# Retention with stacked output products in two chunks, small zero products first, a tile moved ahead of an output, and fewer loads under way

## The reference, cut to what matters

```python
gamma = 1.0 - 2.0 ** (-5.0 - np.arange(H))
Dmat = np.where(rel >= 0, gamma[:, None, None] ** rel, 0.0)       # rel = pos_i - pos_j
attn = np.matmul(q @ k.T / 8 * Dmat, v)                            # per batch and head
x = attn.transpose(0, 2, 1, 3).reshape(1152, 512)
for e in range(4):                                                 # moe: D 512, F 1024
    out += p[:, e:e+1] * (np.maximum(x @ w1[e], 0) @ w2[e])
h = out @ w_in                                                     # 512 -> 2048
y = (h * np.tanh(softplus(h))) @ w_out                             # 2048 -> 512
```

## Time and profile before

| what | value |
|---|---|
| median of 3 runs | 619.76 us (619.45 to 620.73) |
| profiled execution | 620.43 us, of which the span from the first to the last instruction 618.7 us |
| PE busy | 606.0 us, 98% of the span |
| DVE, ACT, POOL busy | 262.9, 234.8, 278.3 us |
| DMA moved | 50.47 MB, mean 82 GB/s |
| mean granted TensorE clock | 0.994 |
| chain that ended last | PE 97%, issue 1%, DVE 1%, DMA 1% |

### The profile page before, as it was taken

The page is one execution under the profiler, slowest core; times in us unless marked ns, Lnnn a source line. Parts: engine busy times, 40 slices in busy tenths (PEclk is TensorE's granted clock), DMA queues, the critical chain, the costliest instruction groups (busy, mean ns, idle before and its releaser), DMA issues.

```text
span 618.7 us, 9829 instructions
## 1 busy us (share of the span) xinstructions
PE 606.0 (98%) x4016; PEld 546.6 (88%) x4016; DVE 262.9 (42%) x361; ACT 234.8 (38%) x434; POOL 278.3 (45%) x230
## 2 busy tenths in 40 slices
PE   7799999999999999999999999999999999999997
PEld 4688999999899999999999999989989999989996
DVE  2468654424254424154534154535545432324334
ACT  2466333322233322223432223435455454334431
POOL 3558645534435545335553435532446543443300
PEclk9799999999999999999999999999999999999999
DMA  8963312322102332012332102321211232201002
GB/s 339 334 218 103 87 41 65 119 84 68 35 35 68 104 103 68 35 35 68 103 88 66 52 34 69 103 68 46 58 34 58 67 101 83 68 1 52 1 1 102
DMA packets 24923, 50.47 MB, mean 82 GB/s; under 512 B 2864, under 2 KB 2992, under 8 KB 24880
## 3 DMA queue, kind: packets, MB, share of 16 engines
q1 hardware_dynamic: 24736, 49.84, 25.5%
q10 hardware_dynamic: 144, 0.02, 0.0%
HBM read 47.49 MB, written 2.36 MB: 81 GB/s over the span
## 4 chain that ended last, share of the span: by engine, by line
PE 97%; issue 1%; DVE 1%; DMA 1%; ACT 0%
PE bank L494 31%; PE bank L496 31%; PE bank L495 31%; PE bank L442 2%; PE bank L470 1%; DMA loaded<-in_first 1%; PE bank L474 1%; PE bank L612 1%; PE bank L447 0%; PE bank L619 0%; DVE acc_sb L889 0%; DVE acc_sb L893 0%; ACT st L686 0%; DVE h_lo L850 0%; ACT h_hi L717 0%
## 5 line engine op out<-in xcount | busy, mean ns | idle before, releaser
L395 POOL TENSOR_TENSOR w_lo<-w_raw,w_hi 128x512 fp32r<-128x512 f32 x96 | 133.9, 1409 | 148.4 <-ACT w_hi L368 144.9
L494 PE MATMUL bank<-w_hi,h_hi 128*128 128x512 f32 x432 | 168.7, 390 | 0.0
L496 PE MATMUL bank<-w_hi,h_lo 128*128 128x512 f32 x432 | 168.4, 390 | 0.0
L495 PE MATMUL bank<-w_lo,h_hi 128*128 128x512 f32 x432 | 168.3, 390 | 0.0
L876 DVE TENSOR_TENSOR h_act<-part,bank 128x384 f32<-128x384 f32 x96 | 52.9, 551 | 170.4 <-PE bank L496 169.9
L390 POOL TENSOR_TENSOR ws<-ws_f,ws 128x1024 fp32r<-128x1024 f32 x24 | 58.4, 2432 | 144.7 <-ACT ws L364 144.7
L496 PEld LDWEIGHTS bank<-w_hi,h_lo 128*128 128x128 f32 x432 | 81.1, 188 | 16.9
L495 PEld LDWEIGHTS bank<-w_lo,h_hi 128*128 128x128 f32 x432 | 81.1, 188 | 12.3
L494 PEld LDWEIGHTS bank<-w_hi,h_hi 128*128 128x128 f32 x432 | 81.0, 188 | 12.1
L722 ACT ACTIVATE part<-bank 128x384 f32<-128x384 f32 x72 | 35.4, 491 | 138.9 <-PE bank L496 138.9
L843 DVE SCALAR_TENSOR_TENSOR h_lo<-h_act,h_hi 128x384 fp32r<-128x384 f32 x64 | 73.4, 1156 | 20.9 <-ACT h_hi L712 20.3
(11 more groups left out here) (88 smaller groups left out, 863.8 us busy)
## 6 DMA issues: line engine op xcount, KB each, us to landing
w_raw<-in_weights SPq DMA_DIRECT2D x144, 256.0 KB, 2.8
loaded<-in_toks SPq DMA_DIRECT2D x9, 512.0 KB, 6.4
loaded<-in_feats SPq DMA_DIRECT2D x8, 512.0 KB, 5.9
out<-acc_sb SPq DMA_DIRECT2D x6, 256.0 KB, 2.0
out<-acc_sb SPq DMA_DIRECT2D x1, 768.0 KB, 3.5
loaded<-in_first SPq DMA_DIRECT2D x1, 726.0 KB, 4.4
ident<-in_ident SPq DMA_DIRECT2D x1, 64.0 KB, 6.0
p_nat<-in_probs ACTq DMA_DIRECT2D x1, 18.0 KB, 6.4
```

Of the source, the lines that this page charges most:

```text
L395: pool.tensor_tensor(w_lo[layer][:, x], w_raw[:, r % RAW], w_hi[layer][:, x].bitcast(F32), ALU.subtract).then_inc(s_wl, 1)
L494: pe.matmul(out, w[0], x[0], start=first, stop=False, **more)
L495: pe.matmul(out, w[0], x[1], start=False, stop=False, **more)
L496: return pe.matmul(out, w[1], x[0], start=False, stop=last, **more)
```

## The change

**Stacked outputs** in chunks 1 and 2 (`STACKED`): state and v stand above one another in the 128 partitions, and q and masked scores too, so that one product over 128 rows replaces two over 64. An output then has 16 products and not 32. For this the host gives feats of these chunks with the halves arranged otherwise, DVE multiplies v of batch 1 by its decay into a tile of its own (`v_decay_again`, `s_va`), POOL's `v_decay` covers half the partitions, the state copy of ACT writes into the place below or above v, and masking is two instructions of 64 partitions. **Zeros:** 60 products of 128x64 by 64 columns (`small_zeros`) stand in place of 7 of 128x512. **Tile 0** runs between `scores_and_state(3)` and `output(3)`; `TILES_IN` then has one tile each at chunks 3 to 6, and two at 7. **Loads:** up to chunk 4 each load waits for an earlier one to land, so that at most three are under way. On DVE, `first_lo(c - 2)` stands ahead of `decayed(c - 1)` in chunks 2 and 3.

```diff
+STACKED = 1, 2
-TILES_IN = {3: (0,), 4: (1,), 5: (2, 3), 6: (4,), 7: (5, 6), 8: (7,)}
+TILE_AMID = {3: 0}
+TILES_IN = {3: (1,), 4: (2,), 5: (3,), 6: (4,), 7: (5, 6), 8: (7,)}
...
-WARM_START, WARM_NEXT = 7, 5
+SMALL, WARM_NEXT = 60, 5
...
+        v_again = sb("v_again", [P, len(STACKED), HEADS, DH])
...
+        def state_and_v(c, b):
+
+            return v_again[:, c - 1] if b else slots[:, c % SLOTS, 2]
+
+        def q_and_masked(c, b):
+
+            return slots[:, c % SLOTS, 1 - b]
...
+            load_feats(1)
             for c in range(1, SLOTS):
-                load_feats(c)
+                feats_there(c - 1)
                 load_toks(c)
+                if c + 1 < SLOTS:
+                    toks_there(c - 1)
+                    load_feats(c + 1)
...
                 sp.wait_ge(s_o, c - SLOTS + 1)
+                if c == SLOTS:
+                    feats_there(c - 1)
                 load_feats(c)
+                if c == SLOTS:
+                    toks_there(c - 1)
                 load_toks(c)
...
                 pe.wait_ge(s_vd, c + 1)
+                if c in STACKED:
+                    pe.wait_ge(s_va, c)
...
+            def of_both(c, b, h):
+                return pe.matmul(ps_o[HALF[h % 2], b, h // 2], state_and_v(c, b)[:, h], q_and_masked(c, b)[:, h],
+                                 start=True, stop=True)
...
+                if c in STACKED:
+                    pe.wait_ge(s_xt, c)
+                    pe.wait_ge(s_st, 2 * c)
+                    pe.wait_ge(s_sm, c + 1)
+                    for hp in range(PAIRS):
+                        for b in range(BATCH):
+                            of_both(c, b, 2 * hp)
+                            mm = of_both(c, b, 2 * hp + 1)
+                    mm.then_inc(s_o, 1)
+                    return
...
+            def small_zeros(count):
+
+                for _ in range(count):
+                    pe.matmul(banks[7][HALF[0], 0:CH], zeros[:, 0:CH], zeros[:, 0:CH], start=True, stop=True)
+
             pe.wait_ge(s_zt, 1)
-            keep_warm(WARM_START)
+            small_zeros(SMALL)
...
                     scores_and_state(c)
+                if c in TILE_AMID:
+                    early_tile(TILE_AMID[c])
                 output(c)
...
+                if c + 1 in STACKED:
+                    act.wait_ge(s_va, c + 1)
                 for b in range(BATCH):
-                    act.activation(st[HALF[b], c % 2], ps_state[HALF[1 - b]], ACT.Copy).then_inc(s_st, 1)
+                    to = state_and_v(c + 1, b)[HALF[1 - b]] if c + 1 in STACKED else st[HALF[b], c % 2]
+                    act.activation(to, ps_state[HALF[1 - b]], ACT.Copy).then_inc(s_st, 1)
...
+            def v_decay_again(c):
+
+                dve.wait_ge(s_toks[c % SLOTS], landed(c))
+                by = key_decay[HALF[1], c].unsqueeze(2).broadcast_to([CH, HEADS, DH])
+                dve.tensor_tensor(v_toks(c, 1), slots[HALF[1], c % SLOTS, 2], by, ALU.mult).then_inc(s_va, 1)
...
+                if 1 < c <= PER_BLOCK:
+                    first_lo(c - 2)
                 if c > 0:
                     decayed(c - 1)
-                if c > 1 and c != PER_BLOCK + 1:
+                if c == 1:
+                    v_decay_again(2)
+                if c > PER_BLOCK + 1:
                     first_lo(c - 2)
```

More of the change, by code:

```diff
@@ L512, in plain_ready, with early_tile @@
                     pe.wait_ge(s_cc, ITEMS * (sums(s) - 1) + (C21, C12)[i] + 1)
+            def early_tile(t):
+                s, i = divmod(t, ITEMS)
+                plain_ready(s, i)
+                plain_products(s, i, range(KT))
             def plain_products(s, i, tiles):
@@ L812, in masked @@
                 dve.wait_ge(s_sc, c + 1)
-                dve.tensor_tensor(masked_scores(c), ps_s[c % SCORES], mask.unsqueeze(1).broadcast_to([P, HEADS, CH]),
-                                  ALU.mult).then_inc(s_sm, 1)
+                if c in STACKED:
+                    for b in range(BATCH):
+                        op = dve.tensor_tensor(masked_scores(c, b), ps_s[c % SCORES][HALF[b]],
+                                               mask[HALF[b]].unsqueeze(1).broadcast_to([CH, HEADS, CH]), ALU.mult)
+                    op.then_inc(s_sm, 1)
+                    return
+                dve.tensor_tensor(slots[:, c % SLOTS, 0], ps_s[c % SCORES],
+                                  mask.unsqueeze(1).broadcast_to([P, HEADS, CH]), ALU.mult).then_inc(s_sm, 1)
+            def v_decay_again(c):
+                dve.wait_ge(s_toks[c % SLOTS], landed(c))
+                by = key_decay[HALF[1], c].unsqueeze(2).broadcast_to([CH, HEADS, DH])
+                dve.tensor_tensor(v_toks(c, 1), slots[HALF[1], c % SLOTS, 2], by, ALU.mult).then_inc(s_va, 1)
             def rows(i):
@@ L1028, in v_decay @@
                 pool.wait_ge(s_toks[c % SLOTS], landed(c))
[L1029 to L1030 removed]
+                rows = HALF[0] if c in STACKED else slice(0, P)
+                v = slots[rows, c % SLOTS, 2]
+                by = key_decay[rows, c].unsqueeze(2).broadcast_to([rows.stop, HEADS, DH])
+                pool.tensor_tensor(v, v, by, ALU.mult).then_inc(s_vd, 1)
             pool.wait_ge(s_feats[0], landed(0))
@@ L1078 @@
     weights = [halves(moe_w1[e], moe_w2[e]) for e in range(MOE_EXPERTS)] + [halves(moe2_w_in, moe2_w_out)]
-    feats = np.stack([by_features(k), by_features(q)], axis=3).reshape(PLACES, P, 2 * KIND)
+    feats = np.stack([by_features(k), by_features(q)], axis=3)
+    for c in STACKED:
+        feats[c] = np.stack([feats[c, 1, :, ::-1], feats[c, 0]])
+    feats = feats.reshape(PLACES, P, 2 * KIND)
     toks = np.stack([by_tokens(v), by_tokens(k)], axis=3).reshape(PLACES, P, 2 * KIND)
```

44 lines of the change are left out of this document (25 added, 19 removed).

## The result

| | before | with the change |
|---|---|---|
| median (11 runs each) | 620.02 us (619.19 to 620.88) | 624.17 us (621.42 to 625.38) |
| profiled execution, its span | 620.43, 618.7 us | 624.44, 622.3 us |
| mean granted clock | 0.994 | 0.989 |

The ratio is 1.0053 (95% interval 1.0042 to 1.0064); the two medians lie 4.15 us apart, 0.67%. So the change is slower by 0.5 to 0.7%, where 617.5 us had been forecast, and the time lies above the forecast's range (615.8 to 620.2).

A forecast was written before the change was run, and what follows sets the result against it. PE, 98% busy, bounds the kernel; only early idle time and slow clock could go. Block times gave 2.0 to 3.5 us gain, idle time 0.6 to 2.1; taking 2.2, 619.76 - 2.2 = 617.5 us, 80% range 615.8 to 620.2.

The forecast's parts named there:

- The reading of the gaps: PE's early issue gaps (2.63, 1.24, 1.53, 0.41 us): PE runs out of program at every 256th instruction, its packet late.
- that rival: Small zeros at the start end late, 107 ns each, 2.5 us late on everything: 620.5 us; chance 0.13.
- The start of tile 0: Ahead of output 3, tile 0 waits for DVE's low half of chunk 2 and starts at 23.0 us.
- The loads held back cost nothing.: Loads up to chunk 4: waiting is free while the DMA engines always have a load waiting.
- About 1 us if the last part lags: Held-back loads: cost about 1 us if the last of a load's 16 parts lags, as when a program packet shares its engine.
- A product over 128 rows holds two quarters: Outputs of chunks 1 and 2: PE time stays 0.9 us each, while 64 records go in each chunk.
- The next has one tile and not two: 38.4, or 39.9 if it is late again.: Later block, at 41.88 us before: one tile, 4.1 us, PE goes on at 38.4, or 39.9 if the packet is late.
- A block costs 4.25 to 5.2 us: Early chunks: each 256-instruction block costs PE at least this while DMA engines are full, so fetch paces chunks without a tile.
- Stacked outputs: Chunks 1 and 2: 128 records fewer, later block starts; DVE's four extra operations of 0.6 to 0.7 us hide.
- the zeros: Start: 106 more records bring the third block's request forward to about 6.5 us; the 2.63 us gap goes.
- Tile 0 ahead of output 3: PE idles 1.8 us before tile 0, yet reaches output(4) at 29.9 us with two tiles done, against 30.83 with one.
- The rival of the rule: Early gaps are not due to instruction count, so fewer and earlier records buy nothing: 619.9 us; chance 0.05.

The follow-up runs named there:

- before_small: Kernel before with 60 small zero products in place of 7 large ones, nothing else: 628.12 us against 620.18, ratio 1.0112.
- loads_free: Changed kernel with the loads issued without waiting, as before the change: 621.89 us against 620.18 for the kernel before, ratio 1.0027.
- free_late_weights: loads_free with the weights behind ident issued only when output 5 is done: 621.20 us against 619.76 for the kernel before, ratio 1.0012.
- small_split: before_small with the weights of chunks 5 to 8 issued half a chunk later: 626.38 us against 620.37 for the kernel before, ratio 1.0089.
- before_held: Kernel before with the change's waits ahead of the loads, nothing else: 621.06 us against 620.18, ratio 1.0013.

## Why the prediction was wrong

**What held.** The reading of the gaps as a program that comes late in blocks of 256 instructions: they moved where the count had put them, near 14 us there is none, and the gap at the last records of `scores_and_state(2)` ended at 18.27 (17.8 forecast). The small zeros took 57 ns each (3.41 us for 60; 53 in before_small with 3.17) and ended ahead of the first load, so that rival fell. (The 0.43 us of a large one is 0.45, 3.17 by seven, and the gaps of 6.3 us are 6.0 by the earlier trace rows; neither changes the forecast.) The start of tile 0 was right for a kernel with free loads (22.97, 23.0 forecast). That there is no gap near 14 was partly luck: two of the three kernels with the same records and free loads have one.

**The step that failed first: "The loads held back cost nothing."** It had a condition, that the DMA engines always have a load waiting and that a load moves within 1.5 us of its issue. From 10.6 to 20.8 us they moved 231 to 284 GB/s, against 399 to 410 with free loads; toks 3 took 6.89 us, not the 4 that three loads of 1.3 us would. "About 1 us if the last part lags" was right in kind and too small, for what it delays was not followed: two weights on SP, then ACT's queue, where a high half of a weight stands ahead of the state copy and of `xa_hi`, then DVE, tile 0, and the whole of tile 0 and `output(3)` at 1.2 GHz. Measured 2.3 us by the medians (loads_free; 1.6 by the ratios), and 0.9 in the kernel before.

**The second: "A product over 128 rows holds two quarters, so 32 passes of it last as long as 64 passes over four quarters: 0.9 us of PE time stay."** That is about right for the output itself (1.15 us for `output(1)` after; 1.1 for an output of 64 passes before, 42.45 to 43.55). But the sum has `scores_and_state(1)` at 1.0 us and puts nothing for what the turned features do to it and to `scores_and_state(0)`: they take 2.0 and 1.9 us, 2 us of PE time more. It put the costs of stacking on DVE, and took PE as unchanged.

**"The next has one tile and not two: 38.4, or 39.9 if it is late again."** In loads_free, free of the waits, PE goes on at 41.80 where before did at 41.88, and its packet lies at 39.4 us, as before at 39.3. All that had been won by then was lost in a gap of 2.20 us, which the double tile had covered before. The forecast had named the mechanism (a burst of loads ahead of the packet) and given it 1.5 us; PE went on 3.4 us later than 38.4.

**"A block costs 4.25 to 5.2 us"** was taken as a price of the block. It is a price of the place. before_small asks for the same blocks of the same work at other moments and has gaps of 3.23, 2.88, 1.78 and 3.56 us. That the loads issued just ahead of the request set it fits free_late_weights (from 4.2 to 1.1 us between the entry and the packet), the one run that holds back nothing but such a burst. But that is one crossing in one trace of each, packets of the same program start up to 2 us apart, the medians don't tell the two apart, and small_split left 6 us of the 8. So this is likely, and not shown. What is shown is the size, up to 8 us by a shift of 106 records, and that it lies in the time until the packet starts.

**"Stacked outputs" and "the zeros"** were costed as parts that hold on their own, with two sums that agreed on 2.0. Both came from one model of the fetch and so could not support one another. Alone, one costs 2.5 us and the other 8. Together with the old tiles and free loads they end at 620.70, no change from before (0.9992 to 1.0018).

**"Tile 0 ahead of output 3"** was included at its gaps (1.8 us idle, one double tile fewer) and expected to come out ahead at the later block. It is a loss of 1.2 to 1.3 us in both kernels in which it was varied alone.

**Outside the span** nothing had been foreseen. Kernels with stacked chunks have 2.1 us there (624.44 - 622.3; 621.81 - 619.7; 622.48 - 620.4), those without 1.8 (621.07 - 619.3; 619.66 - 617.8). The cause is open; it is 0.3 of the 4 us.

**The rival of the rule** gave 619.9 and did not come about: before_small has 11.5 us of gaps at crossings. The page "Runtime: NRT & Kernel Launch" of the Trainium skill, section "Instruction fetch mechanics", calls the cost of a crossing "mostly hidden"; the 11.5 us speak against that for this stretch. The blocks of 256 instructions that the Trainium skill states there agree with the records counted in all sixteen traces.

In terms of the sum, by the medians: loads +2.3 us where 0 had been put, tile +1.2 where it was thought to pay, stacking, zeros and DVE's order together +0.5 (within the noise of 0) where 2 to 3.5 of gain had been put, with what lies outside the span inside these. They add up to 4.0 by the way they are formed, run by run from the changed kernel to the kernel before, so that this is no check of them; by the ratios they are 0.26, 0.22 and 0.05%.

## What to carry to other kernels

Where a profile shows gaps of "issue" at every 256th instruction while loads run, count where the boundaries fall before and after any edit that changes the number of instructions, and measure several shifts of a few dozen cheap instructions: here a shift moved the time from -0.1% to +1.1%, more than any part of the change was meant to bring. An edit that adds or removes instructions can't be judged alone in such a stretch, only beside a run that keeps the count. When data is laid out anew for one product, look at every other product that reads it: here the scores came to share their places in the array with the growth of the state, and took twice the time. And when a load is held back, follow the queue behind it to the end: the weight here was nobody's bound, but a state copy and a high half of x stood behind it on ACT.

## What the runs showed of the hardware that was not expected

- Fewer loads under way move less: 269, 284 and 231 GB/s with at most three of 512 KB (and two weights of 256 KB), 399 to 410 with more, in the same stretches of the same work. In the kernel before the waits do it too (before_held, where the kernel before has 415 in the same stretch):

```profile
10.60:14.00 3.40, 1.73 (x103) 1.46 (x93) 1.85 (x3) 2.54 (x5) 0.88 (x2) 1.00 0.91 313
```

- Two kinds of 64x64 products that read and write the same halves of the partitions take twice the time of two kinds that don't: 2.01 us for 64 matmuls, 0.95 before.
- From the start of a packet of program to PE's going on it takes 2.2 to 2.9 us, in thirteen traces; until it starts, 1.1 to 4.3 us from PE's entry into the block before.
- A hump of 8 us over a shift of 176 records, with the lowest time at 176, 0.1% under that at none.
- Gaps of up to 3.56 us at one boundary, where before had at most 2.63.
- Small products of zeros cost 53 to 57 ns each, the 0.45 us of a large one being 57 for as many columns (3.17 for seven), and behind them the first scores take 1.15 us for 32 matmuls where they took 1.97 before, at a granted clock that reads 1.00 in both.
- 0.3 us more outside the span with stacked chunks, not explained.
